# Attention and MLP: the one-hot expansions of q and k alternate over steps 1 to 4, the first head's sums are taken in step 5

## What is computed

```
q_bits = (q @ proj > 0); k_bits = (k @ proj > 0)      # 6 bits -> one of 64 buckets
mask   = q_bucket[:, None] == k_bucket[None, :]
scores = where(mask, q @ k.T / sqrt(D), -1e9)
attn   = exp(scores - max); attn = attn / (sum(attn) + 1e-9)
x      = attn @ v          # then h = x @ w_in, a rational function of h, @ w_out
                           # then h = x @ w_in2, h - tanh(h), @ w_out2
```

## Time and profile before

| what | value |
|---|---|
| median of three runs | 791.07 us (790.76 to 792.19) |
| the profiled execution's own time | 794.7 us |
| its span | 792.9 us |
| granted TensorE clock, mean over the span | 0.993 |
| TensorE busy | 771.3 us (97%), 3840 matmuls |
| VectorE busy | 554.0 us (70%), 894 instructions |
| ScalarE busy | 476.0 us (60%), 922 |
| GpSimd busy | 127.3 us (16%), 112 |
| attention | 0 to about 245 us; the rest is MLP |

### The profile page before, as it was taken

The page is one execution under the profiler, slowest core; times in us unless marked ns, Lnnn a source line. Parts: engine busy times, 40 slices in busy tenths (PEclk is TensorE's granted clock), DMA queues, the critical chain, the costliest instruction groups (busy, mean ns, idle before and its releaser), DMA issues.

```text
span 792.9 us, 11860 instructions
## 1 busy us (share of the span) xinstructions
PE 771.3 (97%) x3840; PEld 645.7 (81%) x3840; DVE 554.0 (70%) x894; ACT 476.0 (60%) x922; POOL 127.3 (16%) x112
## 2 busy tenths in 40 slices
PE   5979999999999999999999999999999999999998
PEld 3879899989998777877888888888888888888886
DVE  4859999999997999999888988965432322223222
ACT  5859889888887778887666767654432222222221
POOL 5334533543548200000000000000000000000000
PEclk9989999999999999999999999999999999999999
DMA  5766768768563520000000032330000100001001
GB/s 116 157 167 154 163 163 175 172 152 175 120 171 114 159 94 0 1 2 1 0 1 15 26 107 83 103 92 3 0 1 1 53 1 1 0 1 54 0 1 54
DMA packets 64603, 56.54 MB, mean 71 GB/s; under 512 B 31664, under 2 KB 50352, under 8 KB 64560
## 3 DMA queue, kind: packets, MB, share of 16 engines
q1 hardware_dynamic: 62848, 55.52, 28.4%
q10 hardware_dynamic: 1712, 0.46, 0.3%
HBM read 29.57 MB, written 3.19 MB: 41 GB/s over the span
## 4 chain that ended last, share of the span: by engine, by line
PE 75%; DVE 16%; issue 3%; DMA 2%; POOL 2%; SPq 1%; ACT 1%; DVEq 0%; POOLq 0%; ACTq 0%
PE acc L722 28%; PE h_ps L693 27%; PE slot L232 5%; PE turn_ps L354 5%; PE pv_ps L314 4%; PE pv_ps L316 3%; DVE sqr L828 2%; DVE row_min L505 2%; DVE pol L849 2%; DVE pol L841 1%; DVE pt_lo L552 1%; DVE pol L860 1%; DVE pol L835 1%; DVE wout_lo L889 1%; DVE g_lo L873 1%
## 5 line engine op out<-in xcount | busy, mean ns | idle before, releaser
L693 PE MATMUL h_ps<-x_hi,win_lo 128*128 128x512 f32 x384 | 151.6, 395 | 0.0
L693 PE MATMUL h_ps<-x_lo,win_hi 128*128 128x512 f32 x384 | 151.4, 394 | 0.0
L693 PE MATMUL h_ps<-x_hi,win_hi 128*128 128x512 f32 x384 | 151.2, 394 | 0.0
L743 ACT ACTIVATE g_hi<-pol 128x512 fp32r<-128x512 f32 x96 | 60.8, 634 | 129.5 <-PE acc L722 105.2
L873 DVE TENSOR_TENSOR g_lo<-pol,g_hi 128x512 fp32r<-128x512 f32 x96 | 65.9, 687 | 101.2 <-ACT g_hi L743 101.0
L552 DVE TENSOR_TENSOR pt_lo<-turn_ps,pt_hi 128x384 fp32r<-128x384 f32 x192 | 98.0, 551 | 11.2 <-ACT pt_hi L457 9.6
L457 ACT ACTIVATE pt_hi<-turn_ps 128x384 fp32r<-128x384 f32 x192 | 84.0, 490 | 23.7 <-PE turn_ps L354 22.7
L505 DVE TENSOR_REDUCE row_min<-slot 128x1 f32<-128x768 f32 x96 | 90.7, 944 | 7.1 <-PE slot L232 7.1
L433 ACT ACTIVATE E<-slot,row_min 128x768 f32<-128x768 f32 x96 | 87.3, 909 | 2.8 <-DVE row_min L505 2.8
L693 PEld LDWEIGHTS h_ps<-x_lo,win_hi 128*128 128x128 f32 x384 | 72.2, 188 | 17.0
L693 PEld LDWEIGHTS h_ps<-x_hi,win_hi 128*128 128x128 f32 x384 | 72.2, 188 | 16.7
(11 more groups left out here) (105 smaller groups left out, 1364.9 us busy)
## 6 DMA issues: line engine op xcount, KB each, us to landing
win_raw<-in_moe_w_in SPq DMA_DIRECT2D x32, 256.0 KB, 3.1
wout_raw<-in_moe_w_out SPq DMA_DIRECT2D x32, 256.0 KB, 2.8
q_nat<-in_q SPq DMA_DIRECT2D x16, 192.0 KB, 3.5
v_nat<-in_v SPq DMA_DIRECT2D x8, 384.0 KB, 5.4
scale<-softmax_scale SPq DMA_DIRECT2D x16, 192.0 KB, 3.3
qA<-q_hi SPq DMA_DIRECT2D x15, 192.0 KB, 2.5
qB<-q_hi SPq DMA_DIRECT2D x15, 192.0 KB, 2.9
qB<-q_lo SPq DMA_DIRECT2D x15, 192.0 KB, 3.2
```

Source lines behind the costliest of these rows:

```text
L693: mm = eng.matmul(h_ps[t % 4][:, :], w[:, ws], columns(x, kt, c), start=kt + n == 0, stop=kt == KT - 1 and n == 2)
L743: eng.activation(g_hi[:, t % TEMPS, :], pol[:, t % TEMPS, :], ACT.Copy).then_inc(mlp_sems["g_hi"], 1)
```

## The change

`HOT_STEPS` now has the order q half 0, k half 0, q half 1, k half 1 for steps 1 to 4 (before: both q halves, then both k halves). VectorE's second q expansion is therefore made in step 3 instead of step 2, ScalarE's first k expansion in step 2 instead of step 3. The values of `aux_hot` are renumbered to that order. `pe_hot` waits accordingly: a k half for the q half of the same h (`dve_hot(b, h)`), the second q half for the first k half (`act_hot(b, 0)`). The sums and the reciprocal of head 0 are taken in VectorE's step 5 instead of step 4; those of head 1 stay where they are. In pair 0 the expansions are in steps 3 to 6, in pair 7 there are none.

```diff
--- before.py
+++ after.py
@@ -172,7 +172,7 @@
 
 
 
-        HOT_STEPS = {1: (0, 0), 2: (0, 1), 3: (1, 0), 4: (1, 1)}
+        HOT_STEPS = {1: (0, 0), 2: (1, 0), 3: (0, 1), 4: (1, 1)}
         G = T // 2
         GROUPS = TILES // G
 
@@ -191,7 +191,7 @@
             return BIAS + b * AUX_USES + 4 + 1
 
         def aux_hot(b, x, h):
-            return BIAS + b * AUX_USES + 5 + 2 * x + h + 1
+            return BIAS + b * AUX_USES + 5 + 2 * h + x + 1
 
         def act_turn(b, x, h):
             return BIAS + b * AUX_ACT + 2 * x + h + 1
@@ -258,10 +258,8 @@
         def pe_hot(eng, b, x, h):
             if x == 0 and h == 0:
                 eng.wait_ge(sems["aux_dve"], dve_dot(b))
-            elif x == 0:
-                eng.wait_ge(sems["aux_dve"], dve_hot(b, 0))
-            elif h == 0:
-                eng.wait_ge(sems["aux_dve"], dve_hot(b, 1))
+            elif x == 1:
+                eng.wait_ge(sems["aux_dve"], dve_hot(b, h))
             else:
                 eng.wait_ge(sems["aux_act"], act_hot(b, 0))
             eng.matmul(aux_ps[:, 0:HALF], pats[:, 2 * x + h, :], bits[:, :],
@@ -553,7 +551,7 @@
                                       turn_ps[h][:, 0:HALF].rearrange("r (k n) -> r k n", n=P),
                                       pt_hi[dst].bitcast(F32), ALU.subtract
                                       ).then_inc(sems["pt_lo"], 1)
-                if n in (4, 9 if last else 10):
+                if n in (5, 9 if last else 10):
                     dve_scale(eng, p, n // T)
                 if last and n == TILES - 3:
                     dve_step(eng, 0)
```

## The result

The changed kernel takes 799.16 us (median of four runs, 797.46 to 800.47) against 791.07; the ratio is 1.0087, with a 95% interval of 1.0066 to 1.0108. That is 8.1 us slower, where 2.6 had been forecast, and beyond the range that was given.

A forecast was written before the change was run, and what follows sets the result against it. The end of VectorE's x_sum of step 6 was taken to set the pair's length. 5 x 0.45 for middle pairs, 0.2 for pair 6 and 0.15 for pair 7 gave 2.6 us: 791.07 + 2.6 = 793.7, range 791.0 to 796.4.

The forecast's parts named there:

- (e): Addition in step 5 meets GpSimd's x_lo, loses next to nothing; x_sum of step 6 0.40 to 0.51 later, taken as 0.45.
- (g): SyncE's queue: scale_out waits for step 5's reciprocal, delaying copies; k copy at 133.7, needed at 134.03: costs nothing, slim cover.
- (a): VectorE's second q expansion, 0.52 us, leaves step 2 for step 3, so VectorE is ready for x_sum of step 3 at 119.41.
- (b): ScalarE's first k expansion ahead of pv_low in step 2: x_sum of step 3 gains 0.24, not 0.52; VectorE idles 0.28.
- (c): VectorE's steps 3 to 6: pt_lo of step 5 waits for pt_hi until about 124.72, a second idle stretch of some 0.2.
- (d): Sums now in step 5: x_sum of step 6 at 126.98, 0.51 later; the sums' time itself neutral.
- the lock bites: Rival, 12%: x_lo holds the sums in step 5 until 126.4; +1.0 per pair, 796.4 us in all.
- (h): Other pairs: pair 0 nothing, with 0.5 either way, behind its 4.18 us wait; pair 6 0.2; pair 7 0.15.
- (f): TensorE's second k product in step 4 waits for the q expansion: nothing to 0.1, absorbed before x_sum of step 6.
- narrow span: Total of 792.9 to 794.7 us, with every pair at 0.3 or 0.6 and pair 0 at its ends.

The follow-up runs named there:

- e6: Kernel before with the second q expansion moved behind x_sum of step 6 and the k copy issued ahead of the q copy: 790.44 us, ratio 0.9964.
- e5: Changed kernel with head 0's sums in step 7 and scale_out behind load_v and the copies of the expansions: 790.39 us, ratio 0.9975.
- e3: Changed kernel without the addition of 1e-9 to the row sums, the reciprocal reading them directly: 794.83 us, ratio 1.0029 to the kernel before.
- e10: e8 with head 0's sums in step 7 and scale_out behind both copies of the expansions: 789.42 us, ratio 0.9972 to the kernel before.
- e4: Changed kernel with head 0's scale_out behind load_v and the copies of the expansions in SyncE's order: 794.65 us, ratio 1.0034 to the kernel before.
- e1: Kernel before with only head 0's sums moved from step 4 to step 5: 798.80 us, ratio 1.0075.
- e7: Kernel before with head 0's scale_out behind load_v and the copies of the expansions in SyncE's order: 791.72 us, ratio 0.9982.
- e2: Changed kernel with head 0's sums back in step 4, leaving only the new order of the expansions: 795.59 us, ratio 1.0033 to the kernel before.
- e8: e6 with SyncE's order split copies, load_v, k copy, scale_out, q copy, scale_in: 789.58 us, ratio 0.9958 to the kernel before.
- e9: e8 without the addition of 1e-9 to the row sums: 788.99 us, ratio 0.9952 to the kernel before.
- e11: The kernel of e8 measured a second time without any edit: 789.04 us, ratio 0.9961 to the kernel before.

## Why the prediction was wrong

The sign was right, and in the middle pairs the place and the mechanism; the size was not, pair 1 was not foreseen, and 799.16 lies outside 791.0 to 796.4. Two steps failed, (e) and (g).

(a), (b), (c) held: x_sum of step 3 moved by 0.24, VectorE got the two idle stretches, all beginnings up to pt_lo of step 5 are within 0.08 of the working. That x_sum of step 6, and not that of step 3, sets the pair, the changed kernel shows itself: x_sum of step 3 came 0.24 earlier and the pair is 0.78 longer. e6 shows it from the other side: 0.52 of work taken out between step 0 and step 6 made the pair 0.38 shorter.

(d) with its 0.51 held too, as far as it goes. e5 takes the sums out of the stretch and has pairs of 28.73. Put back at the 0.40 that they take when nothing holds them, they give an estimate of 29.13 for the change without the hold, 0.54 above 28.59; the other 0.24 of the 0.78 is put down to the held addition, which is 0.29 longer. e3 takes out the addition alone and arrives at the same 28.74: its reciprocal stands in the stretch, but from pt_lo of step 5 to x_sum of step 6 it is 1.87 us there and 1.86 in e5.

**(e) is the first step that failed.** It said that the addition would find x_lo all but finished and lose nothing to it. The mechanism was the right one, but x_lo's end was reckoned with the 5.18 us of pair 6, which has its GpSimd instructions closer together, although the pair in question showed its own x_lo ending at 124.53 + 1.84 = 126.37, 0.6 later than the working had it. In the changed kernel it is the 5.56 shown above; from x_norm's assumed beginning at 120.6 that gives x_lo's end at 126.16 (measured 126.11 on this scale) and a hold of 0.3 us (measured 0.29). The lower bound of 0.40 had been borrowed from pair 6 in the same way: row_min 0.14 behind the addition is how pair 6 spaces them, not what a held addition brings (it is 0.14 there in e10 too, where nothing held it), and in pair 3 it is 0.23 after a held one as well. So a middle pair grew by 0.78 and not by 0.45; x_sum of step 6 came 0.79 later. The case "the lock bites", given 12% at 1.0 per pair, is the one that came, 0.2 cheaper than priced, since GpSimd's x_norm, and with it x_lo, began some 0.25 earlier, behind the earlier x_sum of step 3.

The Trainium skill, page "SBUF — State Buffer", section "Who interferes with whom", has the shared pair held for a whole instruction, and lets a VectorE instruction with at most one SBUF input outside the two-port modes pass. The trace agrees with both. Wherever the addition was held, by up to 1.65 us, it ended 0.02 to 0.04 us behind the GpSimd instruction. pt_lo, whose one SBUF input is pt_hi, kept its 1.02 inside x_lo, and the reciprocal of e3, which the section's list of instructions that take the shared pair does not have, passed.

**(g) is the second.** It said "nothing, with a slim cover" for SyncE's later queue. For the pairs 2 to 5 that is so (the k copy takes 4.4 to 5.6 us there, and TensorE does not wait for it). In pair 1 it took 7.7, outside the 3.9 to 6.5 that the trace of before had, and the pair grew by 2.2 us more than the others. The worst landing of before (6.5) had been in pair 1 as well; issued at 71.08 it would have been there at 77.6, when TensorE had been waiting since 76.9. The median was taken for a pair that had its own row. e4 shows that the wait goes when scale_out stands behind the copies. e1 shows that scale_out in front is not enough to bring it: with the same order and as late an issue its copy landed in 4.9. What makes the landing 7.7 in pair 1 of the changed kernel and of e3, and in no other, stays open. In both the profile counts an instruction-fetch packet on the DMA engines while the copy is on its way (between 74 and 76 us, and between 72 and 74), but so it does in e5 and e7 (between 68 and 70), where the copy landed in 4.9 and 5.1.

(h) pair 6 and pair 7 came out as said to 0.2. Pair 0 was taken as a fixed wait of 4.18 us. It is not fixed: x_sum of step 6 of pair 0 begins anywhere between 32.9 and 35.3 us in the traces (33.01, 34.55 and 35.28 in e5, e4 and e7, with one order of the queue), and the later TensorE comes, the less it waits; the landing itself comes 1.6 us earlier with the copies first. (f) had said nothing to 0.1: the weight load before the second k product waited 0.20 for the q expansion, ahead of the longer wait of step 6. The narrow span of 792.9 to 794.7 is six pairs at 0.3 and at 0.6; the 0.5 of pair 0 that it names is not in it.

**The sum.** By the trace the change costs 5.7 us, 3.1 more than the forecast: 1.7 from the middle pairs (5 x 0.35), 2.2 from the copy in pair 1, less 0.5 in pair 0 and some 0.3 in the rest. By the medians it costs 8.1. The profiled execution of before lay 3.6 over its median, that of the changed kernel 1.3 over its own, and the prediction took the stretches concerned to be the same in both. The three runs behind 791.07 were on the low side: 66 later runs of the kernel before have medians of 791.6 to 793.0, against which the change costs 6.2 to 7.6. That did not decide the outcome, as 5.7 on 791.07 is 796.8 and outside the range too. The traces differ by up to 2.8 us in what the clock does behind the wait of pair 0 (last section); whether runs of one kernel differ by the same was not measured.

## What to carry to other kernels

When a piece of work is moved so that a wait becomes shorter, add up the work up to the next wait of the same kind as well: if the engine was busy without a gap in between, the time comes back there, and only work taken out of the whole stretch is a gain. A tiny instruction is not cheap if it can be held by another engine; look at what that engine does at the new place, in the very pair and not in a similar one. And an issue that waits in a queue delays all that stand behind it, so a transfer that nobody is waiting for belongs behind those that somebody is (here it took 1.6 us off the landing in pair 0).

## What was not expected of the hardware

An addition of 128x6 numbers took 0.16 us in free places and up to 1.81 us (e7) when GpSimd was at work. After it had been held, the reciprocal began 0.12 to 0.14 us behind its end in the loop's pairs, as in the free case, and 0.02 to 0.04 in the pairs 6 and 7, held or free.

After TensorE's wait of 3.55 us in pair 0 the granted clock was at half (1.2 GHz) and then partly so; these are two stretches of the changed kernel, the third number from the right being the clock:

```profile
44.00:48.00 4.00, 3.49 (x12) 3.42 (x13) 0.96 (x1) 0.00 (x0) 0.62 (x1) 0.50 1.05 250
48.00:52.00 4.00, 4.00 (x25) 3.80 (x27) 2.34 (x5) 2.67 (x6) 0.22 (x1) 0.69 0.52 118
```

The kernel before has the same behind its wait of 4.18 us, so this is no effect of the change:

```profile
44.00:48.00 4.00, 2.91 (x10) 2.84 (x11) 0.96 (x1) 0.00 (x0) 1.31 (x2) 0.51 1.05 260
48.00:52.00 4.00, 4.00 (x20) 3.96 (x20) 2.22 (x5) 2.35 (x5) 0.02 (x1) 0.64 0.51 123
```

In e7, where that wait was 0.63 us, it stayed at 2.4 GHz:

```profile
44.00:48.00 4.00, 4.00 (x30) 3.88 (x28) 2.98 (x7) 2.91 (x8) 0.00 (x0) 1.00 0.58 152
48.00:52.00 4.00, 4.00 (x29) 3.00 (x28) 3.37 (x7) 2.92 (x8) 0.00 (x0) 1.00 0.98 215
```

What it costs can be read from the scores of step 9, where the wait ends, to x_sum of step 0 of pair 1, which is the same work in all of them (but for one addition, which e3 and e9 leave out). It is 7.7 us in e4, e7 and e10, whose waits were 0.95, 0.63 and 0.77 us; 9.0 to 9.3 in e2, e3, e5, e6, e8, e9 and e11, with waits of 2.35 to 4.20; and 10.3 to 10.5 in before, changed and e1, with 3.55 to 4.22. So a long wait there cost 1.3 to 2.8 us beyond its own length. The wait of 1.90 us in pair 1 had no such consequence: the stretch from 76 to 80 us was granted in full, and from those scores to step 0 of pair 2 it took 7.7 us.
